# Where the second half of w_in is folded in, and which ScalarE work stands ahead of it, in a three-stage layer kernel (attention, soft MoE, feed-forward)

## The reference

```
attn_out = windowed_attention(q, k, v)      # 4 batches, 8 heads, 576 tokens, head width 64, window 128
x = attn_out as [2304, 512]

logits = x @ phi                            # 2304 x 32 slots (8 experts, 4 slots each)
d = softmax(logits, axis=0);  slot_input = d.T @ x
for e in range(8):
    h = maximum(slot_input[e] @ w1[e], 0.0) # 512 -> 1024
    slot_out[e] = h @ w2[e]                 # 1024 -> 512
c = softmax(logits, axis=1)
x = c @ slot_out                            # 2304 x 512

h = x @ w_in                                # 512 -> 2048
g = h * clip(h + 3.0, 0.0, 6.0) / 6.0
out = g @ w_out                             # 2048 -> 512
```

## Time and profile before

| | us |
|---|---|
| median of 3 runs | 451.93 (451.76 to 452.66) |
| profiled execution, its time | 451.76 |
| profiled execution, its span | 450.0 |
| PE busy in the span | 417.5 (93%) |
| DVE / ACT / POOL busy | 233.7 / 212.7 / 70.1 |
| the part before the w1 products (from the start) | 172.8 |
| w1 products to the last w2 product | 172.8 to 214.1 |
| last stage | 214.1 to 450.0 |

### The profile page before, as it was taken

How to read it: one execution, slowest core, us unless ns; L and a number is a source line. 1 busy time by engine, 2 the same in 40 slices (tenths; PEclk the granted TensorE clock), 3 DMA queues, 4 the chain that set the end, 5 groups by cost and what they waited for, 6 DMA issues and landing times.

```text
span 450.0 us, 10183 instructions
## 1 busy us (share of the span) xinstructions
PE 417.5 (93%) x3764; PEld 341.0 (76%) x3764; DVE 233.7 (52%) x698; ACT 212.7 (47%) x601; POOL 70.1 (16%) x112
## 2 busy tenths in 40 slices
PE   3899999999999958887697999999999999999996
PEld 2688888878888844567475888888888888888885
DVE  2466686777678756040345534444354434454442
ACT  2788776878787710000635434343333434343431
POOL 1133133223223302000656000000000000000000
PEclk9999999999999986998998999999999999999999
DMA  9759898898797482999910100001010101010101
GB/s 179 190 149 259 225 260 218 236 260 230 202 286 189 132 311 86 387 386 396 396 55 1 40 7 23 25 0 47 0 47 0 47 0 47 0 47 0 47 1 48
DMA packets 75494, 61.41 MB, mean 136 GB/s; under 512 B 57792, under 2 KB 57792, under 8 KB 75456
## 3 DMA queue, kind: packets, MB, share of 16 engines
q1 hardware_dynamic: 75456, 60.89, 44.9%
HBM read 56.16 MB, written 4.72 MB: 135 GB/s over the span
## 4 chain that ended last, share of the span: by engine, by line
PE 86%; DVE 5%; ACT 4%; issue 3%; DMA 1%; SPq 0%; DVEq 0%
PE probs_turned L958 23%; PE out_turned L958 22%; PE scores L757 7%; PE probs_turned L766 4%; PE scores L901 4%; PE out_turned L782 4%; PE scores L940 4%; PE scores L886 3%; PE routes L812 3%; PE out_turned L786 3%; PE turns L740 2%; PE turns L797 2%; ACT probs L397 2%; PE turns L732 2%; PE routes L836 1%
## 5 line engine op out<-in xcount | busy, mean ns | idle before, releaser
L683 DVE SCALAR_TENSOR_TENSOR g<-u,scores 128x512 f32<-128x512 f32 x72 | 49.5, 688 | 109.7 <-ACT u L435 109.7
L440 ACT ACTIVATE g_hi<-g 128x512 fp32r<-128x512 f32 x72 | 45.5, 632 | 119.8 <-PE out_turned L958 119.1
L397 ACT ACTIVATE probs<-probs,rowmin 128x128 f32<-128x128 f32 (+1 forms) x160 | 62.0, 391 | 3.5 <-DVE rowmin L508 3.5
L958 PE MATMUL probs_turned<-w_out_hi,g_hi 128*128 128x512 f32 x144 | 57.5, 399 | 5.4 <-ACT g_hi L440 5.0
L958 PE MATMUL probs_turned<-w_out_lo,g_hi 128*128 128x512 f32 x144 | 57.1, 396 | 0.0
L958 PE MATMUL out_turned<-w_out_hi,g_hi 128*128 128x512 f32 x144 | 57.0, 396 | 0.0
L958 PE MATMUL out_turned<-w_out_lo,g_hi 128*128 128x512 f32 x144 | 56.9, 395 | 0.0
L958 PE MATMUL out_turned<-w_out_hi,g_lo 128*128 128x512 f32 x144 | 56.8, 394 | 0.0
L958 PE MATMUL probs_turned<-w_out_hi,g_lo 128*128 128x512 f32 x144 | 56.6, 393 | 0.0
L689 DVE TENSOR_TENSOR g_lo<-g,g_hi 128x512 fp32r<-128x512 f32 x72 | 53.1, 738 | 1.9 <-ACT g_hi L440 1.9
L435 ACT ACTIVATE u<-scores 128x512 f32<-128x512 f32 x72 | 41.9, 582 | 2.1 <-PE scores L940 2.1
(11 more groups left out here) (131 smaller groups left out, 627.2 us busy)
## 6 DMA issues: line engine op xcount, KB each, us to landing
weight_ring<-in_moe_w_dram SPq DMA_DIRECT2D x32, 1024.0 KB, 7.5
out_dram<-y SPq DMA_DIRECT2D x18, 256.0 KB, 2.0
q_in<-in_q_dram SPq DMA_DIRECT2D x16, 256.0 KB, 4.3
k_in<-in_k_dram SPq DMA_DIRECT2D x16, 256.0 KB, 4.6
v_in<-in_v_dram SPq DMA_DIRECT2D x16, 256.0 KB, 3.8
weight_ring<-in_moe_w_in_dram SPq DMA_DIRECT2D x8, 512.0 KB, 12.4
weight_ring<-in_moe_w_out_dram SPq DMA_DIRECT2D x4, 1024.0 KB, 15.5
q_in<-in_q_dram SPq DMA_DIRECT2D x4, 128.0 KB, 4.0
```

The source lines that it names most:

```text
L397: act.activation(probs[0:R, m % 2, h, :], probs[0:R, m % 2, h, :], ACT.Exp, bias=rowmin[0:R, m % 2, h:h + 1], scale=-1.0, accum_out=rsum[0 ...
L440: act.activation(g_hi[:, p % 2, :], g_sb[:, p % 4, :], ACT.Copy).then_inc(ghi_ready, 1)
L683: dve.scalar_tensor_tensor(out=g_sb[:, p % 4, :], in0=u_sb[:, p % 2, :], scalar=6.0, in1=bank[p % 4], op0=ALU.min, op1=ALU.mult).then_inc( ...
L958: ins = pe.matmul(bank[4 + kk][:, :], g[:, p % 2, cols], w[:, c, :], start=(p == 0 and i == 0 and a == 0), stop=(p == FPAIRS - 1 and i == ...
```

## The change

Four edits, none of which changes what is computed:

1. DVE: the maximum over the slots of each token (`rmax`, L619) stands ahead of the copy to `slot_masked` (L615) and no longer behind it.
2. ACT: copy_wp(1) and relu(0) stand ahead of split_high(0) and split_high(1).
3. PE: only hidden(0) and hidden(1) stand ahead of the first chunk; hidden(2) and (3) stand ahead of project(0) and project(1). compact(1), spread_wp(2) and spread_wp(3) all stand ahead of project(3), with hidden(4) and (5) behind them.
4. DVE: split_compact(1) stands at n = 3, just ahead of copy_wp(2), and no longer at n = 2.

```diff
-            split_high(0)
-            split_high(1)
             copy_wp(1)
             relu(0, 0)
+            split_high(0)
+            split_high(1)
             chunk(0, False)
...
+            link(dve.tensor_reduce(rmax[:, 0, :], logits[:, :, :], AX.X, ALU.max))
...
             dve.tensor_copy(own_slots(slot_m, KC, 0, KC), bank[3][:, 0:P].rearrange(
                 "p (c e s) -> p e c s", c=KC, s=SPE)).then_inc(slot_ready, 1)
-            link(dve.tensor_reduce(rmax[:, 0, :], logits[:, :, :], AX.X, ALU.max))
...
-                    if isinstance(m, int) and n == 2:
+                    if isinstance(m, int) and n == 3:
                         split_compact(1)
-                    if isinstance(m, int) and n == 3:
                         copy_wp(2)
...
-                    if first and p == 1:
+                    if first and p == 3:
                         compact(1)
-                    if first and p == 2:
                         spread_wp(2)
                         spread_wp(3)
-                    if first and p == 3:
                         hidden(4, 0, 4)
-                        hidden(5, 0, 5)
-                    if first and p < 4:
+                    if first and p == 2:
                         pass
                     elif p + 2 < FPAIRS:
                         hidden(n + 2, m, p + 2)
...
-            for p in range(PARTS):
-                hidden(p, 0, p)
+            hidden(0, 0, 0)
+            hidden(1, 0, 1)
             chunk(0, False)
```

More of the change, by code:

```diff
@@ L465, in copy_wp @@
                 act.activation(wp[:, n * WCOLS:(n + 1) * WCOLS], wp_bank(n), ACT.Copy).then_inc(wp_ready[1], 1)
+            copy_wp(1)
+            relu(0, 0)
             split_high(0)
             split_high(1)
-            copy_wp(1)
-            relu(0, 0)
             chunk(0, False)
```

## The result

| | before | after |
|---|---|---|
| median | 451.85 us (4 runs, 451.16 to 452.66) | 457.28 us (4 runs, 456.95 to 457.64) |
| profiled execution, time and span | 451.76, 450.0 | 456.89, 455.2 |
| PE busy | 417.5 | 419.4 |

The changed kernel is slower by a ratio of 1.0119 (95% interval 1.0103 to 1.0137), 5.4 us.

What follows compares the result with a forecast made beforehand. PE was taken to bound the kernel, so only the delay of the first chunk before PE's steady run counted. Terms -1.23 + 4.60 + 0.15 = +3.5 us gave 455.3 on the profiled run, 455.4 as median; range 454.0 to 457.3.

Steps and rivals of the forecast that it cites:

- Edit 1: At the slot copy on DVE: it starts 0.20 us later, +0.15 us at the end; bounds 0 and +0.81.
- project(0): Start of project(0) on PE: 224.45 in place of 222.88, +1.57 us; its end at 228.4, +0.95 us.
- project(2): Start of project(2) on PE, waiting for g_lo(2): 231.85 in place of 233.08, -1.23 us.
- The chain to project(3): From the end of project(2) to project(3): four serial links, 8.15 us in place of 3.55, +4.60 us.
- The race with POOL: At low(3) on DVE: POOL's step again costs it 1.1 us; if the race turns, 454.3 us, chance 0.12.
- The rival that it isn't slower: At ACT's splits: late w_out landings make the change gain, 451.9 us or less; chance 0.04 together with a covered chain.
- The slow stretches: PE at 1.2 GHz behind its stalls: two before, two after, about 1.7 us each; one more, 456.0 to 457.1, chance 0.2.
- The forecast's own narrow range: End time with the forecast's small uncertainties, 454.8 to 456.0 us, chance 0.6.
- the wide one: Range of the end time reaching over the race turned and the extra slow stretch: 454.0 to 457.3 us.

Runs made afterwards that it cites:

- the experiment: Changed kernel with split_high(5) moved on ACT from n = 3 to n = 4, so POOL has no work when low(3) starts: 455.39 us.
- edits 3 and 4 alone: Kernel before with only the moves on PE and of split_compact(1) on DVE, ACT and the maximum as before: 456.49 us, ratio 1.011.
- the changed kernel with low(3) first: Changed kernel with high(3) ahead of copy_wp(3) on ACT and low(3) ahead of copy_wp(2) and gate(4) on DVE: 453.12 us.

## Why the prediction was right, and where it was off

- **Edit 1**: +0.2 us at the slot copy was said, +0.17 measured; nothing of it can be seen in the time. Right.
- **project(0)**: 6.68 us from the zero forecast, 6.65 measured. high(0) behind four splits, low(0) held by POOL's second step: 1.02 us, from 223.85 to 224.87, against 224.35 minus 223.35 forecast. The start was right. Its length was not: 3.95 us forecast, with the clock back at 227.1, and 4.41 measured (224.97 to 229.38), with the clock back at about 228.7.
- **project(2)**: 14.08 forecast, 14.05 measured. The number was right by luck. The forecast had PE wait 0.45 us here for g_lo(2). In the trace project(1) ran 0.4 us later than forecast (11.29 from the zero, 10.88 forecast), because project(0) took longer, and project(2) followed it without a wait; g_lo(2) took 0.68 us and was done 0.2 us earlier from the zero than forecast (at 232.07). PE itself was the bound, and the two errors cancelled.
- **The chain to project(3)**: 8.15 us from the end of project(2) forecast. In the trace compact(1) starts at 235.22 and project(3) at 243.39: 8.17. All four links stood as written: 2.00 (235.22 to 237.22), 2.06 (to 239.28), 1.01 (to 240.29), 3.10 (to 243.39). Right.
- **The race with POOL**: the same loser by the same 0.05 us (241.47 and 241.52). Right, and the experiment confirms its price of 1.1 us.
- **The rival that it isn't slower** was rightly given little.
- **The slow stretches**: this is the term that failed, in its size. "The slow stretches: two before, two after" was the step. After has the clock down from within the pause to the end of project(3), so that project(3) takes 5.68 us to the next in place of 4.59: +1.1. The forecast gave that 0.2 and 456.0 to 457.1 as its price. It came in both traces that could show it: those with the whole pause of 3.04 us and no matmuls in it (the changed kernel, edits 3 and 4 alone) have 5.68 and 5.50 us from project(3) to project(4); with POOL out of the way and a pause of 1.95 us it is 4.62.
- **The baseline**: one slow stretch of the profiled execution, in project(0), was taken as fixed. Five of six traces with before's pause don't have it; all with the change's pause do. That is worth up to 1.6 us in a trace and, by the groups of executions, some 0.9 us in the time, and it was in no term.
- **The first 218 us**: the zero lay 0.55 us later than in before. It lies between 217.8 and 219.6 in all the kernels without an edit there and without a lost race, so this is within the spread between executions and is not put down to the change.

Together, on the two profiled executions: 3.47 (chain) + 1.09 (project(3) at the lower clock) + 0.55 (the zero) = 5.1 of the 5.2 us between the spans. The forecast's own narrow range, 454.8 to 456.0, was missed; the wide one holds because it left room for the slow stretch, with 0.02 us to spare.

## What to carry to other kernels

Before work is gathered into one place of a queue, follow the circle from the last instruction that feeds the slot to the first that needs it: each hop there is a whole latency, and the sum of four such hops was predicted here to 0.02 us from the instructions' own rows. When a wait ends on an instruction that stands behind another in its queue, as low(3) behind gate(4), try the other order first: that alone gave 1.9 us by the medians and some 4 by the traces. With the next pair too and POOL's memset it was 4.2 by the medians, but nothing more by the traces. And a pause of PE can be paid again in the clock behind it: look at several executions for how often the clock falls, since one trace may be the exception.

## What the runs showed of the hardware

**Matmuls of no use made a kernel faster**, by 2.0 to 2.5 us for 20 of them: the granted clock stayed at 1.00 where it was 0.50.

**VectorE and GpSimd can shut each other out at another place than expected.** In the trace of edits 3 and 4 alone (and again in that of the changed kernel with low(3) first) slot_in, which takes 0.31 us elsewhere, ends only with POOL's memset:

```profile
171.67 2.08 DVE L605 TENSOR_SCALAR slot_in<-slot_acc,rtot 128x128 f32<-128x128 f32 x1
171.84 1.83 POOL L351 MEMSET hid_masked<- 128x2080 f32 x1
```

In the nine other traces with this pair, with the same 0.16 to 0.17 us between the two starts, slot_in takes 0.31 us, and the memset 1.91 in place of the 1.83 that it takes where it was held back and has no neighbour: there, it seems, POOL is the one that waits, by 0.08 us. Here DVE starts first by the record and still waits until POOL is done. It cost these executions some 1.8 us at the first expert's product; taken out of the kernel before, it doesn't show in the median. How often it is lost, and in which kernels, two traces of eleven don't tell. The Trainium skill (SBUF — State Buffer, "Who interferes with whom") says that tensor_scalar can use both port pairs and then contends with GpSimd, while an instruction with two SBUF inputs contends only with a GpSimd instruction that reads SBUF. Both cases are in these traces: slot_in against a memset that only writes, and low against POOL's subtraction, 1.77 us against 0.69. The page's sentence that issue order decides who blocks agrees with low(3), which starts 0.05 us behind POOL's step and loses; for slot_in the recorded starts have the loser ahead.

**A gap of 0.91 us inside compact(0)**, put down to issue, stands in the changed kernel's trace and in nine others, always behind the second matmul, while the DMA engines are full. The four traces without it (before among them) are those in which the last w2 products just ahead of it ran at the lower clock: PE comes later and isn't stopped. In these traces, then, PE doesn't keep the time that it wins there, and what it waits for isn't settled by these runs.
